# Earlier load and cast of a third weight piece, a gate in the first block, and loads queued ahead of the moves of y, in a recurrence with two MLPs

## The chip, the cores and the metric

The kernel runs on one core of one Trainium2 chip. The metric is the device time in microseconds of one execution; lower is better. The core's engines are TensorE (PE, matmul), VectorE (DVE), ScalarE (ACT), GpSimd (POOL) and SyncE (SP), which here only issues DMAs.

## What is computed

```python
f = 1.0 / (1.0 + np.exp(-f_logit))                  # B 4, H 8, S 768, D 48
for t in range(S):
    state = f[:, :, t, :, None] * state + einsum('bhd,bhe->bhde', k[:, :, t], v[:, :, t])
    y[:, :, t] = einsum('bhd,bhde->bhe', q[:, :, t], state)
x = y.transpose(0, 2, 1, 3).reshape(3072, 384)
x = (sigmoid(x @ w_gate) * (x @ w_val)) @ w_out     # d_ff 1536
h = x @ w_in                                        # d_ff 2048
out = (h * sigmoid(1.702 * h)) @ w_out2
```

All in float32.

## The kernel before

**Three stages that overlap.** The recurrence is cut into 48 units, each of 256 tokens and one pair of heads; four units (numbers 4s to 4s+3) make a step of 256 tokens. The first MLP works on 7 groups of tokens: two of 256 columns, five of 512. Each group has 12 blocks j of 128 hidden columns. The second MLP has 6 groups of 512 with 16 blocks. Every float32 product is made of three matmuls, from a rounded part (hi) and a rest (lo) of each operand: ScalarE's copy makes hi, a subtraction on DVE makes lo. That holds for x (x_hi, x_lo), the hidden activations (act_hi, act_lo) and the weights (w_hi, w_lo).

**What a block does.** PE makes the gate product in `up_ps` bank 0 (`hidden`), then the value product in bank 1, then, where a visit stands, the recurrence's matmuls (`visit`), then the output product of the block before (`out`). ScalarE takes the sigmoid of the gate (L634), DVE multiplies with the value (L823), ScalarE rounds to act_hi (L640), DVE makes act_lo (L832). PE's gate product of block q waits for the sigmoid of block q-1 (`sig_done`), the value product for its mul (`mul_done`).

**Units.** For unit n: SP or ScalarE loads f, SP loads q, k and v. `forget(n)` on ScalarE makes the gates (L545, L546); `prepare(n)` on DVE makes the running product and its inverse (L722, L726); `decay(n)` on POOL makes q_dec (L474) and k_dec (L479). A visit is one turn of PE for up to three units: (turned, kept, made). `turned` gets its scores, `kept` its state update, `made` its y. After it ScalarE copies k and y out of PSUM (`take_k` L564, `take_y` L570), and SP moves y into `x_raw` with two or three DMAs (`move_y` L369). In the blocks from unit 6 on, made = turned - 2.

**Order by hand.** Which block has which visit, gate and prepare is written in tables. In group 0 visits stand at blocks 1, 2, 4, 6, 8, in groups 1 to 5 at 0, 1, 3, 4, 5, 7, 8, 9. Prepares of groups 1 to 5 stand at 0, 2, 3, 4, 6, 7, 10, 11. With a the first turned unit of a group (5 for group 0, 10, 18, 26, 34, 42 for the others), the n-th visit turns unit a+n, and the n-th prepare of a group after 0 is of unit a+n+2. At block 10 (`SPLIT_AT1`) ScalarE runs `x_first_part` for the next group, three casts, one per slab of 128 rows of x (L584), and DVE `x_second_part` (L769). The cast of a slab waits until the y of the units that fill it have been moved (`y_moved`). The third slab needs all units of the group. These are complete with the unit made at block 9. On DVE the prepare at block 10 stands ahead of `x_second_part`.

**Waits of the loads.** `load_f(n)` waits for the gate of unit n-2, `load_kq(n)` for q_dec of n-2 before the two loads of q, and for k_dec of n-2 before those of k. `load_v(n)` waits for the visit that made unit n-4. All SP issues stand in one program, in order.

**Weights of the first MLP.** `load_w1(t)` on ScalarE's queue brings piece t (576 KB) into one of four places, `w1_first_part(t)` is its cast (L526), `w1_second_part(t)` the subtraction on DVE (L776), at block t-2. Piece 0 is split by POOL (L486). Before the first block eight visits have run.

The functions that the change touches, and what calls them:

Of the kernel before, what the change touches and what calls it, by code (L numbers as in the profile page):

```python
# [16 lines left out]
def gla_moe_moe2(nc, q_t, k_t, f_t, v_n, v_t, w1, w2, out_t, x_dram, x2_dram):  # L17
# [51 lines left out]
    ahead_of = VISITS[BEFORE_MLP][0]  # L69
    for g in range(NG1 - 1):  # L70
        if g == 0:
            forgets = {j: n + 3 for n, j in enumerate((1, 2, 4, 6, 8))}
            prepares = {j: n + 1 for n, j in enumerate((0, 1, 3, 5, 7, 9))}
        else:
            forgets = {j: n + 3 for n, j in enumerate((0, 1, 3, 4, 5, 7, 8, 11))}
            prepares = {j: n + 2 for n, j in enumerate((0, 2, 3, 4, 6, 7, 10, 11))}
        FORGET_AT.update({(g, j): ahead_of + n for j, n in forgets.items()})
        PREPARE_AT.update({(g, j): ahead_of + n for j, n in prepares.items()})
        ahead_of += len(forgets)
    SPLIT_AT1 = 10  # L80
    SPLIT_AT2 = 4
    AHEAD = 3
# [1 line left out]
    with ExitStack() as ctx:  # L84
# [9 lines left out]
        def wait(eng, s, value):  # L94

            if value > 0:
                eng.wait_ge(s, value)
# [120 lines left out]
        def pieces_of_pair(p):  # L218

            pieces = []  # L220
            for i in range(PAIR):
                at, end = (PAIR * p + i) * D, (PAIR * p + i + 1) * D
                src = 64 * i
                while at < end:
                    m = min(end, (at // P + 1) * P) - at
                    pieces.append((slice(src, src + m), at // P, slice(at % P, at % P + m)))
                    src, at = src + m, at + m
            return pieces
# [3 lines left out]
        def moves(s, n):  # L232

            return sum(MOVES[m % UG] for m in range(s, n, YS))
# [100 lines left out]
        with nc.Block() as block:  # L335

            @block.sync
            def _(sp):
                def load_f(n):
                    if n < UNITS:  # L340
                        u = Unit(n)
                        sp.wait_ge(gate_done, n - 1)
                        for i in range(PAIR):
                            sp.dma_start(f_raw[rows[i], u.s, :], f_t[u.pair, i, :, u.tokens]).then_inc(f_loaded[u.s], 16)

                def load_kq(n):
                    if n < UNITS:
                        u = Unit(n)
                        wait(sp, q_dec_done, n - 1)
                        for i in range(PAIR):  # L350
                            sp.dma_start(q_raw[rows[i], u.s, :], q_t[u.pair, i, :, u.tokens]).then_inc(q_loaded[u.s], 16)
                        wait(sp, k_dec_done, n - 1)
                        for i in range(PAIR):
                            sp.dma_start(k_raw[rows[i], u.s, :], k_t[u.pair, i, :, u.tokens]).then_inc(k_loaded[u.s], 16)

                def load_v(n):
                    if n < UNITS:
                        u = Unit(n)
                        if n >= 4:
                            sp.wait_ge(visit_done, out_visit[n - 4] + 1)  # L360
                        sp.dma_start(v_raw[:, n % 4, :, :],
                                     v_n[u.pair, :, u.third * BLOCKS:(u.third + 1) * BLOCKS, :]).then_inc(v_loaded[n % 4], 16)

                def move_y(n, pieces=slice(None)):
                    u = Unit(n)
                    sp.wait_ge(y_taken, n + 1)
                    wait(sp, x_split, u.group * KC)
                    for src, slab, dst in pieces_of_pair(u.p)[pieces]:
                        sp.dma_start(x_raw[dst, slab, u.in_group], y_t[src, n % YS, :]).then_inc(y_moved[n % YS], 16)  # L369
# [14 lines left out]
                def load_w2(t):  # L384
                    if t >= STAGED:
                        sp.wait_ge(w2_split, t - STAGED + 1)
                    sp.dma_start(w2_stage[:, t % STAGED, :], w2[:, t * PIECE2:(t + 1) * PIECE2]).then_inc(w2_loaded[t % STAGED], 16)
# [13 lines left out]
                move_y(1)  # L401
                move_y(2, slice(0, 2))
                move_y(3, slice(1, None))
                for n in range(4, 8):
                    load_v(n)
                load_kq(6)
# [3 lines left out]
                for q in range(BLOCKS1):  # L410
                    b = BLOCK[q]
                    if b.j == 1 and b.g:
                        store(b.g - 1)
                    if (b.g, b.j) in VISIT_AT:
                        turned, _, made = VISITS[VISIT_AT[b.g, b.j]]
                        if made is not None:
                            move_y(made)
                            load_v(made + 4)
                        if turned is not None:
                            load_kq(turned + 3)  # L420
                            load_f(turned + 4)
                    if b.g == NG1 - 2 and b.j == J1 - 1:
                        for t in range(STAGED):
                            load_w2(t)
                    if b.g == NG1 - 1 and b.j == 2:
                        load_x2(0)
                        for t in range(STAGED, J2):
                            load_w2(t)
# [86 lines left out]
            def _(act):  # L515
                def load_w1(t):

                    if t >= 4:
                        wait_w1(act, t - 4)
                    act.dma_start(w1_staged(t), w1[:, t * PIECE1:(t + 1) * PIECE1]).then_inc(w1_loaded[t % 4], 16)  # L520

                def w1_first_part(t):

                    act.wait_ge(w1_loaded[t % 4], 16 * (t // 4 + 1))
                    piece = slice(t * PIECE1, (t + 1) * PIECE1)
                    act.copy(w_hi[:, piece], w1_staged(t)).then_inc(w1_hi_done, 1)  # L526
# [8 lines left out]
                def forget(n):  # L535
                    if n >= UNITS:
                        return
                    u = Unit(n)
                    act.wait_ge(f_loaded[u.s], (u.uses + 1) * 32)
                    if n < 2:  # L540
                        act.wait_ge(gaps_set, 5)
                    wait(act, scan_done, n - 1)
                    f_c = f_raw[:, u.s, :].rearrange("p (c t) -> p c t", c=CH)

                    act.activation(gate[:, u.s, :].rearrange("p (c t) -> p c t", c=CH)[:, :, 1:C], f_c[:, :, 1:C], ACT.Sigmoid)  # L545
                    act.activation(floor[:, u.s, :].rearrange("p (c t) -> p c t", c=CH)[:, :, 0], f_c[:, :, 0],  # L546
                                   ACT.Sigmoid).then_inc(gate_done, 1)

                def first_move_y(n, pieces):
                    u = Unit(n)  # L550
                    act.wait_ge(y_taken, n + 1)
                    for src, slab, dst in pieces_of_pair(u.p)[pieces]:
                        act.dma_start(x_raw[dst, slab, u.in_group], y_t[src, n % YS, :]).then_inc(y_moved[n % YS], 16)

                def first_load_f(n):
                    u = Unit(n)
                    wait(act, gate_done, n - 1)
                    for i in range(PAIR):
                        act.dma_start(f_raw[rows[i], u.s, :], f_t[u.pair, i, :, u.tokens]).then_inc(f_loaded[u.s], 16)
# [6 lines left out]
                def take_y(n):  # L566
                    u = Unit(n)
                    act.wait_ge(visit_done, out_visit[n] + 1)
                    wait(act, y_moved[n % YS], 16 * moves(n % YS, n))
                    act.copy(y_t[:, n % YS, :].rearrange("p (c r t) -> p c r t", c=BLOCKS, r=SIDES),  # L570
                             banks(out_visit[n])[:, :, Y_COL:Y_COL + BLOCKS * C].rearrange("p r (c t) -> p c r t", c=BLOCKS)).then_inc(y_taken, 1)
# [36 lines left out]
                forget(4)  # L608
                take_y(1)
                first_load_f(6)  # L610
                forget(5)
                w1_first_part(1)
                take_y(2)
                first_move_y(2, slice(2, None))
                take_y(3)
                first_move_y(3, slice(0, 1))
                first_load_f(7)
                load_w1(2)
                take_k(4)
                x_first_part(0)  # L620
                load_w1(3)
                w1_first_part(2)
                load_w1(4)
                forget(6)
                forget(7)

                for q, b in enumerate(BLOCK):
                    if b.first_mlp:
# [12 lines left out]
                    if b.first_mlp and (b.g, b.j) in VISIT_AT:  # L641
                        turned, _, made = VISITS[VISIT_AT[b.g, b.j]]
# [455 lines left out]
```

## Time and profile before

| | |
|---|---|
| device time, three runs | 968.01, 969.16, 1051.86 us; median 969.16 |
| profiled execution | 968.01 us, its span in the trace 966.2 us |
| granted TensorE clock, mean | 0.992 |
| busy: PE, DVE, ACT, POOL | 98%, 51%, 31%, 11% |

One run in three was far above the other two, which agree within 0.15%. The profiled execution is the fastest one. All rows below are of its span. Times are in microseconds from the span's start unless ns is written. PE's durations overlap, since matmuls are pipelined; the distance from one start to the next is what a matmul costs.

### The profile page before, as it was taken

The page shows a single profiled execution, that of the slowest core. Times are in us where ns is not written, and L with a number is a line of the kernel's source. Part 1 is how long each engine was busy: PE and PEld are TensorE (multiplying, and loading weights), DVE is VectorE, ACT ScalarE, POOL GpSimd, SP SyncE. Part 2 cuts the span into 40 slices and gives each one's busy share as a digit, 9 for nine tenths or more (in the row PEclk, how much of TensorE's full clock was granted, in tenths as well). Part 3 has the DMA queues.
Part 4 walks back from the last instruction along what each step waited for, and adds up shares of the span by engine and source line. Part 5 has one row for each costly group of instructions (what it writes and reads, how often), then busy time and mean ns, then how long its engine had stood idle before and what let it go on. Part 6 is the DMA issues. An engine that isn't in the chain of part 4 may idle for free.

```text
span 966.2 us, 17729 instructions
## 1 busy us (share of the span) xinstructions
PE 948.8 (98%) x7159; PEld 789.7 (82%) x7159; DVE 491.9 (51%) x876; ACT 303.7 (31%) x621; POOL 106.9 (11%) x125
## 2 busy tenths in 40 slices
PE   8899999999999999999999999999999999999997
PEld 5799988888888888888788888888888888888886
DVE  8897876547555664565333234344343443443433
ACT  3453332223222222322224333323332233333322
POOL 4211211101110111111003440000000000000000
PEclk9899999999999999999999999999999999999999
DMA  5652322112111211121022330020020100100000
GB/s 152 204 167 61 83 63 67 53 51 66 52 46 42 82 45 50 33 76 28 24 104 66 98 115 1 0 66 1 1 66 1 55 12 1 66 1 1 33 1 35
DMA packets 44005, 52.33 MB, mean 54 GB/s; under 512 B 8464, under 2 KB 33808, under 8 KB 43920
## 3 DMA queue, kind: packets, MB, share of 16 engines
q1 hardware_dynamic: 41056, 43.20, 15.4%
q10 hardware_dynamic: 2864, 7.95, 2.8%
q8 instruction: 59, 0.97, 0.4%
q14 instruction: 26, 0.21, 0.1%
HBM read 36.96 MB, written 9.44 MB: 48 GB/s over the span
## 4 chain that ended last, share of the span: by engine, by line
PE 90%; DVE 4%; issue 2%; DMA 1%; SPq 1%; ACT 1%; ACTq 0%; POOL 0%; DVEq 0%
PE up_ps L975 16%; PE up_ps L977 16%; PE up_ps L976 16%; PE out_ps L975 12%; PE out_ps L977 11%; PE out_ps L976 11%; PE att_ps L968 3%; PE att_ps L935 2%; PE att_ps L957 1%; DMA stage<-w 1%; PE turn_ps L914 1%; PE att_ps L947 1%; DVE w_lo L776 1%; DMA k_raw<-k_t 1%; DVE act_lo L832 0%
## 5 line engine op out<-in xcount | busy, mean ns | idle before, releaser
L975 PE MATMUL up_ps<-x_hi,w_hi 128*128 128x512 f32 (+1 forms) x792 | 294.2, 372 | 3.6 <-ACT act_f L634 3.0
L977 PE MATMUL up_ps<-x_hi,w_lo 128*128 128x512 f32 (+1 forms) x792 | 293.8, 371 | 0.0
L976 PE MATMUL up_ps<-x_lo,w_hi 128*128 128x512 f32 (+1 forms) x792 | 293.7, 371 | 0.0
L975 PE MATMUL out_ps<-act_hi,w_hi 128*128 128x512 f32 (+1 forms) x540 | 207.9, 385 | 0.7 <-DVE act_lo L832 0.7
L977 PE MATMUL out_ps<-act_hi,w_lo 128*128 128x512 f32 (+1 forms) x540 | 202.9, 376 | 0.0
L976 PE MATMUL out_ps<-act_lo,w_hi 128*128 128x512 f32 (+1 forms) x540 | 202.6, 375 | 0.0
L640 ACT CAST act_hi<-act_f 128x512 fp32r<-128x512 f32 (+1 forms) x180 | 106.5, 592 | 253.0 <-DVE act_f L823 180.7
L832 DVE TENSOR_TENSOR act_lo<-act_f,act_hi 128x512 fp32r<-128x512 f32 (+1 forms) x180 | 118.1, 656 | 113.7 <-ACT act_hi L640 113.7
L975 PEld LDWEIGHTS up_ps<-x_hi,w_hi 128*128 128x128 f32 x792 | 150.0, 189 | 30.0 <-issue 3.6
L976 PEld LDWEIGHTS up_ps<-x_lo,w_hi 128*128 128x128 f32 x792 | 150.1, 190 | 25.3
L977 PEld LDWEIGHTS up_ps<-x_hi,w_lo 128*128 128x128 f32 x792 | 150.1, 189 | 25.2
L826 DVE TENSOR_TENSOR act_f<-act_f,up_ps 128x512 f32<-128x512 f32 x96 | 66.0, 687 | 173.4 <-ACT act_f L636 173.4
L823 DVE TENSOR_TENSOR act_f<-act_f,up_ps 128x512 f32<-128x512 f32 (+1 forms) x84 | 51.1, 608 | 163.0 <-PE up_ps L977 159.5
L975 PEld LDWEIGHTS out_ps<-act_hi,w_hi 128*128 128x128 f32 x540 | 101.6, 188 | 22.2 <-DVE act_lo L832 1.2
L636 ACT ACTIVATE act_f<-up_ps 128x512 f32<-128x512 f32 x96 | 57.4, 598 | 192.9 <-PE up_ps L977 192.9
L977 PEld LDWEIGHTS out_ps<-act_hi,w_lo 128*128 128x128 f32 x540 | 101.6, 188 | 18.7
L976 PEld LDWEIGHTS out_ps<-act_lo,w_hi 128*128 128x128 f32 x540 | 101.7, 188 | 17.3
L634 ACT ACTIVATE act_f<-up_ps 128x512 f32<-128x512 f32 (+1 forms) x84 | 45.0, 535 | 176.8 <-PE up_ps L977 176.8
L726 DVE RECIPROCAL inv_prod<-prod 128x256 f32<-128x256 f32 x48 | 84.1, 1753 | 1.7
L474 POOL TENSOR_TENSOR q_dec<-q_raw,prod 128x256 f32<-128x256 f32 x48 | 35.2, 734 | 317.5 <-DVE prod L722 263.6
L752 DVE SCALAR_TENSOR_TENSOR state<-state,p_end 128x48 f32<-128x48 f32 x176 | 47.4, 269 | 6.2
L479 POOL TENSOR_TENSOR k_dec<-k_raw,inv_prod 128x256 f32<-128x256 f32 x48 | 37.8, 788 | 50.1 <-issue 41.0
(68 smaller groups left out, 511.7 us busy)
## 6 DMA issues: line engine op xcount, KB each, us to landing
stage<-w SPq DMA_DIRECT2D x16, 384.0 KB, 3.2
stage<-w ACTq DMA_DIRECT2D x9, 576.0 KB, 4.4
q_raw<-q_t SPq DMA_DIRECT2D x96, 48.0 KB, 1.9
k_raw<-k_t SPq DMA_DIRECT2D x96, 48.0 KB, 1.9
v_raw<-v_n SPq DMA_DIRECT2D x48, 96.0 KB, 2.2
x_raw<-x_dram SPq DMA_DIRECT2D x6, 768.0 KB, 4.5
out_t<-final SPq DMA_DIRECT2D x18, 256.0 KB, 2.3
f_raw<-f_t SPq DMA_DIRECT2D x80, 48.0 KB, 1.9
```

Source lines behind the costliest of these rows:

```text
L479: pool.tensor_tensor(k_dec[:, u.s, :], k_raw[:, u.s, :], inv_prod[:, u.s, :], ALU.mult).then_inc(k_dec_done, 1)
L634: act.activation(act_f[:, b.t, 0:b.n], up_ps[:, 0, 0:b.n], ACT.Sigmoid).then_inc(sig_done, 1)
L636: act.activation(act_f[:, b.t, 0:b.n], up_ps[:, b.j % 2, 0:b.n], ACT.Sigmoid, scale=1.702).then_inc(sig_done, 1)
L640: act.copy(act_hi[:, b.t, 0:b.n], act_f[:, b.t, 0:b.n]).then_inc(act_hi_done, 1)
L726: dve.reciprocal(inv_prod[:, u.s, :], prod[:, u.s, :]).then_inc(inv_done, 1)
L752: dve.scalar_tensor_tensor(out=after[:, c, :], in0=state_before(u, c), scalar=p_end[:, n, c:c + 1], in1=after[:, c, :], op0=ALU.mult, op1= ...
L823: dve.tensor_tensor(act_f[:, b.t, 0:b.n], act_f[:, b.t, 0:b.n], up_ps[:, 1, 0:b.n], ALU.mult).then_inc(mul_done, 1)
L826: dve.tensor_tensor(act_f[:, b.t, 0:b.n], act_f[:, b.t, 0:b.n], up_ps[:, b.j % 2, 0:b.n], ALU.mult).then_inc(mul_done, 1)
L832: dve.tensor_tensor(act_lo[:, b.t, 0:b.n], act_f[:, b.t, 0:b.n], act_hi[:, b.t, 0:b.n].bitcast(F32), ALU.subtract).then_inc(act_split, 1)
L975: pe.matmul(dst, w_hi[:, at:at + P], m_hi, start=first, stop=False)
L976: pe.matmul(dst, w_hi[:, at:at + P], m_lo, start=False, stop=False)
L977: return pe.matmul(dst, w_lo[:, at:at + P], m_hi, start=False, stop=last)
```

## The change

It does four things. It adds unit 7 to the gates of group 0's blocks (at block 0) and takes it out of the sequence before the first block; the other gates keep their blocks. It issues the load of the third piece of w1 on ScalarE right behind the load of f for unit 6, and casts it before the copy of k of unit 4 (`take_k(4)`) instead of after the casts of x; the cast of the second piece goes behind the copy of y of unit 2. The load of f for unit 7 is issued by SP. And in the blocks SP issues the loads of f and of q and k ahead of the moves of y and the load of v, where it was the other way round.

```diff
-            forgets = {j: n + 3 for n, j in enumerate((1, 2, 4, 6, 8))}
+            forgets = {j: n + 2 for n, j in enumerate((0, 1, 2, 4, 6, 8))}
...
-        ahead_of += len(forgets)
+        ahead_of += 5 if g == 0 else 8
...
                 move_y(3, slice(1, None))
+                load_f(7)
                 for n in range(4, 8):
                     load_v(n)
...
                         turned, _, made = VISITS[VISIT_AT[b.g, b.j]]
+                        if turned is not None:
+                            load_f(turned + 4)
+                            load_kq(turned + 3)
                         if made is not None:
                             move_y(made)
                             load_v(made + 4)
-                        if turned is not None:
-                            load_kq(turned + 3)
-                            load_f(turned + 4)
...
                 first_load_f(6)
+                load_w1(2)
                 forget(5)
-                w1_first_part(1)
                 take_y(2)
                 first_move_y(2, slice(2, None))
+                w1_first_part(1)
                 take_y(3)
                 first_move_y(3, slice(0, 1))
-                first_load_f(7)
-                load_w1(2)
+                w1_first_part(2)
+                load_w1(3)
                 take_k(4)
                 x_first_part(0)
-                load_w1(3)
-                w1_first_part(2)
                 load_w1(4)
                 forget(6)
-                forget(7)
```

## Rows read from the trace of the kernel before

**Rows 1.** The page, busy us, share of the span, instructions by engine.

```profile
PE 948.8 (98%) x7159; PEld 789.7 (82%) x7159; DVE 491.9 (51%) x876; ACT 303.7 (31%) x621; POOL 106.9 (11%) x125
```

**Rows 2.** Stretches: us; busy of PE, PEld, DVE, ACT, POOL; clock, DMA share, GB/s.

```profile
23.00:24.00 1.00, 0.99 (x13) 0.85 (x14) 0.96 (x2) 0.62 (x2) 0.61 (x1) 0.50 0.03 4
...
31.20:34.10 2.90, 0.01 (x1) 0.04 (x1) 0.89 (x4) 2.23 (x6) 0.72 (x1) 0.84 0.99 298
34.10:40.00 5.90, 5.90 (x53) 5.45 (x54) 5.87 (x8) 3.04 (x8) 1.46 (x2) 0.50 0.77 234
...
140.00:470.00 330.00, 327.34 (x3147) 266.47 (x3150) 192.40 (x368) 88.53 (x211) 43.72 (x58) 1.00 0.18 51
```

**Rows 3.** Waits between 27 and 82 us: who for whom, us, times, longest.

```profile
PE up_ps L975 <- ACT act_f L634: 3.0, 1, 3.0
...
DVE act_f L823 <- ACT act_f L634: 2.0, 1, 2.0
```

**Rows 4.** Timelines of ScalarE and DVE at the start: start, duration, instruction [idle before].

```profile
19.41 0.79 ACTq L559 DMA_DIRECT2D f_raw<-f_t  x2
...
26.44 0.45 ACTq L520 DMA_DIRECT2D stage<-w  x1
...
31.72 1.15 ACT L526 CAST w_hi<-stage 128x1152 fp32r<-128x1152 f32 x1 [2.99 <-DMA stage<-w]
...
33.59 0.36 ACT L634 ACTIVATE act_f<-up_ps 128x256 f32<-128x256 f32 x1
...
31.56 0.41 DVE L734 TENSOR_TENSOR scores<-att_ps,causal 128x256 f32<-128x256 f32 x1
```

**Rows 5.** The chain that ended last, 20 to 82 us: start, duration, what.

```profile
34.40 0.51 DVE w_lo L776
...
79.25 0.33 DVE act_f L823
...
79.63 0.38 PE up_ps L975
```

**Rows 6.** Waits of SP's queue, 140 to 480 us, and of ScalarE, 80 to 470.

```profile
SPq L351 <- POOL q_dec L474: 22.5, 3, 7.8
...
ACT gate L545 <- DMA f_raw<-f_t: 7.6, 5, 2.2
```

**Rows 7.** Timeline of the boundary of groups 2 and 3, all engines.

```profile
212.01 1.98 SPq L369 DMA_DIRECT2D x_raw<-y_t  x2
...
219.28 1.66 ACT L584 CAST x_hi<-x_raw 128x512 fp32r<-128x512 f32 x3
...
221.60 0.78 SPq L351 DMA_DIRECT2D q_raw<-q_t  x2
222.05 0.60 ACT L634 ACTIVATE act_f<-up_ps 128x512 f32<-128x512 f32 x1 [1.10 <-PE up_ps L977]
...
223.72 0.78 SPq L354 DMA_DIRECT2D k_raw<-k_t  x2
224.54 0.89 SPq L344 DMA_DIRECT2D f_raw<-f_t  x2
...
225.70 0.39 PE L977 MATMUL out_ps<-act_hi,w_lo 128*128 128x512 f32 x1
225.93 0.39 PE L975 MATMUL up_ps<-x_hi,w_hi 128*128 128x512 f32 x1
```

**Rows 8.** The same of groups 1 and 2.

```profile
131.48 1.16 SPq L369 DMA_DIRECT2D x_raw<-y_t  x2
...
136.59 0.47 PE L975 MATMUL up_ps<-x_hi,w_hi 128*128 128x512 f32 x1 [0.26 <-DVE x_lo L769]
...
137.06 0.78 SPq L354 DMA_DIRECT2D k_raw<-k_t  x2
...
137.63 0.49 PE L975 MATMUL up_ps<-x_hi,w_hi 128*128 128x512 f32 x1
```

**Rows 9.** The page, DMA issues: count, KB each, median us from issue to landing.

```profile
x_raw<-y_t SPq DMA_DIRECT2D x71, 48.0 KB, 2.0
```

## The prediction, on record before the changed kernel was built

> **What bounds the kernel now.** I read the page's busy shares first [rows 1]: PE is busy 98% of the span and DVE 51%, so in most of the run nothing can be won or lost except by making PE stand still. The table of stretches [rows 2] says where PE does stand still: 327.3 of 330 us busy between 140 and 470, at full clock (2.4 GHz), but 0.01 of 2.9 us in 31.2 to 34.1, and in the 5.9 us after that it works all the time at a granted clock of 0.50 (1.2 GHz). So the start holds the one real stall, 3.0 us.
>
> The waits of 27 to 82 us name it [rows 3]. PE waited 3.0 us for ScalarE's sigmoid of block 0 and DVE 2.0 us for the same. ScalarE's timeline [rows 4] shows why: it issued the load of the third piece at 26.44 and stood 3.0 us ahead of its cast, until 31.72; then came the gates of units 6 and 7, and only at 33.59 the sigmoid. PE had by 31.2 ended both products of block 0 [rows 2].
>
> The chain that ended last [rows 5] then says who is the bound behind the stall. From 34.40 to 79.25 it runs on DVE alone (mul, w_lo, act_lo, prod, inverse, states, and "issue"), and goes over to PE at 79.63. In this first group DVE and PE have nearly the same work, and DVE is the later one.
>
> **The change part by part. The start.** The third load is issued behind the load of f for unit 6, at 19.41 + 0.79 = 20.2 instead of 26.44 [rows 4]. DMA then is busy with the second piece, but in 23 to 24 us its share is 0.03 [rows 2], so the third should be in by about 25, at worst 26. That is an estimate: 5.3 us as the same load took before (26.44 to 31.72). Its cast needs 1.15 us and takes the place of idle time, as ScalarE has little to do before the casts of x. The gate of unit 7 goes behind block 0's act_hi, where ScalarE waits for DVE over long stretches. Left ahead of the sigmoid is one gate (0.6 us), so the sigmoid is set by PE's gate product. DVE then comes to block 0's mul when its own earlier work ends, at 31.56 + 0.41 = 32.0 instead of 34.0: 2.0 us, which is its whole idle time before that mul. PE's stall and its half clock go, 3.0 plus about half of 5.9, but since DVE is the bound up to 79 us, PE keeps only DVE's 2.0. The rest comes back as small waits of PE for DVE. **Term 1: -2.0 us.** Bounds: -2.3, if the pauses between DVE's instructions shrink too; and +1.0, if the earlier and the fourth load, now beside the moves of y for units 2 and 3, delay the third slab of x by 3 us (that load took 5.3 us against the 2 us of a move [rows 4, 9]). The load of f for unit 7 goes to SP, 0.9 us in front of four loads of v that are needed 5 us later: nothing.
>
> **Gates and f loads in the blocks.** Only unit 7's gate moves; the later ones keep their blocks. The loads of f and q/k now stand ahead of move_y and load_v. ScalarE waited 7.6 us in five places of 80 to 470 us for f [rows 6], and these waits go. PE waited for none of them: it was busy 327.3 of 330 us [rows 2], and what is left lies in the visits. So this is worth 0.
>
> **What the new order on SP costs.** SP's queue is in order: whatever waits holds what is behind it. So for every visit I asked what load_f(turned + 4) and load_kq(turned + 3) wait for, and whether that comes before the y of the same visit is taken. load_f waits for the gate of unit turned + 2, made in an earlier block in every case. load_kq waits for q_dec and k_dec of unit turned + 1, so for DVE's prepare of that unit. In group 0 the prepares of blocks 0, 1, 3, 5, 7 come before the visits of 1, 2, 4, 6, 8. In groups 1 to 4 all come before too, except one: the visit of block 9 needs the prepare that stands at block **10**. (In group 5 the visit of block 9 has no turned unit.) These are the long waits of SP [rows 6]: 22.5 us in three places of 140 to 480 us, 7.8 at the longest. Today they are harmless, because the move of y and the load of v went out first. After the change the moves of the last unit of the next group stand behind them, and x_first_part, which ScalarE runs at block 10, waits for these moves at its third slab. ScalarE is in order as well: behind it stands the sigmoid of block 11, and PE cannot begin the next group without that.
>
> The boundary of groups 2 and 3 in numbers [rows 7]. Today: the moves at 212.01, x_hi at 219.28, sigmoid of block 11 at 222.05. After: q loads, released by q_dec, at 221.60, k loads, released by k_dec, 223.72 to 224.50. There the f loads stood (224.54), and now the two moves do. The second is issued 0.58 later (two took 1.16 at the other boundary [rows 8]), at 225.12, and lands 2.0 us later [rows 9], at 227.1. The cast of the third slab takes 0.53, the sigmoid 0.60, the signal 0.1: PE can begin at 228.4. Today it begins the next group at 225.93 [rows 7]. Stall: **2.5 us**, between 2.2 and 2.7 for landings of 1.8 to 2.2. The boundaries behind groups 3 and 4 have the same pattern (with this one they are the three waits of [rows 6], about 7.5 us each), so three times: 7.5 us.
>
> The boundary of groups 1 and 2 [rows 8], where blocks are 256 wide and PE is through sooner: k loads from 137.06 to 137.84, moves from 137.88, the second at 138.46, landed at 140.5, cast until 141.0, sigmoid of 256 columns 0.4, PE at 141.5. Today PE starts at 136.59 and, after two short waits for x_lo, runs through from 137.63, its fourth matmul; three take 0.69, so it stands as if started at 136.9. Stall: **4.6 us**, 4.3 to 4.9. **Term 2: 4.6 + 7.5 = +12.1**, bounds 10.9 and 13.0.
>
> **The clock.** The trace has one comparable case: after 3.0 us without a matmul the granted clock was 0.50, and 5.9 us of work ran at it [rows 2], where half was lost: 2.95. For the stall of 4.6 I take these 2.95. For the three of 2.5, shorter than the row, the bounds are 0 and 2.95; I take the middle, 1.5, as the stall is nearer to 3.0 than to the waits of 0.3 that left the clock alone. **Term 3: 2.95 + 3 x 1.5 = +7.5**, bounds 2.95 and 11.8. "TensorE: Matmul & The Clock Gate" of the Trainium skill, section "HAM oscillation — how this bites in real kernels", tells of a kernel in which every wait for a load between two bursts puts the clock back to half. [...]
>
> **Sum:** -2.0 + 12.1 + 7.5 = +17.6 us. The profiled execution took 968.0 (span 966.2), 1.2 below the median of 969.2; the sum gives 985.6 on the one and 986.8 on the other. I say 986.
>
> **Rivals.**
> 1. The stalls are there but the shorter ones leave the clock alone: -2.0 + 12.1 + 2.95 = +13.1, 981. For it: the clock was still full in the first part of the 2.9 us (0.84 in the mean [rows 2]). Chance 0.17.
> 2. All four stalls cost the clock fully: -2.0 + 12.1 + 11.8 = +21.9, 990. Chance 0.15.
> 3. The move isn't held, or comes early enough: then only term 1 is left, 966 to 967, not slower. That would need SP to pass the wait, or PE to have 2.5 us of slack at the boundary; [rows 7] show a matmul every 0.23 us up to 225.93 and none. "DMA: Bandwidth & Descriptors" of the Trainium skill, section "Anatomy of one DMA — SWDGE (gpsimd) path", says that DMA engines don't wait on semaphores and the issuing sequencer does, ahead of dispatch. By that the move can't pass; the rows agree: SP's queue stood 7.8 us for q_dec [rows 6] with nothing passing. Were it otherwise, this rival's 967 would be the result. Chance 0.10.
> 4. The start doesn't win: the x slab is late or the third piece lands after 26.3. Then +1.0 instead of -2.0 and 989 with the rest. It decides if the moves of y for unit 3 land later than about 28, when the third slab is cast today. Chance 0.08.
>
> **How the numbers follow.** Forecast 0.50, rivals as above. Range 974 to 993: below, all low bounds give +9.3 (977), and a little is left for stalls partly hidden; above, rival 2 with the upper bound of the moves, 992. It leaves out rival 3 and a tail. A measurement of this kernel can tell about 2%, 19.4 us, so the line is at 988.5. Over it lie rival 2, most of rival 4 and a tenth of the forecast: 0.27. Faster by over 2% would need a gain that no row has: 0.01. Within: 0.72.
>
> **What the profile after would show.** Right: ScalarE's x_hi at block 10 of groups 1 to 4 with a wait for DMA x_raw<-y_t between the second and third slab, of some 5 to 7 us; PE waits for ScalarE's act_f L634 of about 4.6 once and 2.5 three times; SP's move after the k loads; half clock behind at least the first; at the start no wait for stage<-w, PE's 3.0 gone and DVE's chain at 79 us about 2.0 earlier. Wrong, if the moves go out before the q loads at block 9, if ScalarE's x_hi doesn't wait, or if group 0 gives back much more than 2.0, which would mean that DVE wasn't its bound.

## The result and the profile after

The changed kernel took 981.45 us (median of 6 runs, 980.36 to 983.54) against 969.16 us for the kernel before: a ratio of 1.013, 95% interval 1.0112 to 1.0148. The 969.16 are the median of five runs; a sixth, of 1051.86 us, is a slow one and is left out. The change makes the kernel slower by 1.3%, 12.3 us, where 986 was said. The profiled executions have spans of 966.2 and 980.4 us, 14.2 apart.

The quickest way to see where 14.2 us came in is one instruction that each group has once: ScalarE's first cast of x at block 10. First the kernel before, ScalarE's timeline around the six places (start, duration, instruction, idle before):

```profile
79.92 1.02 ACT L584 CAST x_hi<-x_raw 128x256 fp32r<-128x256 f32 x3
...
132.89 1.75 ACT L584 CAST x_hi<-x_raw 128x512 fp32r<-128x512 f32 x3
...
308.57 1.66 ACT L584 CAST x_hi<-x_raw 128x512 fp32r<-128x512 f32 x3
...
397.85 1.66 ACT L584 CAST x_hi<-x_raw 128x512 fp32r<-128x512 f32 x3
...
486.48 1.66 ACT L584 CAST x_hi<-x_raw 128x512 fp32r<-128x512 f32 x3
```

The one of group 2, at 219.28, stands in [rows 7]. The same of the changed kernel, where the line is L585:

```profile
78.50 1.01 ACT L585 CAST x_hi<-x_raw 128x256 fp32r<-128x256 f32 x3
...
131.48 1.14 ACT L585 CAST x_hi<-x_raw 128x512 fp32r<-128x512 f32 x2
...
139.06 0.62 ACT L585 CAST x_hi<-x_raw 128x512 fp32r<-128x512 f32 x1 [6.45 <-DMA x_raw<-y_t]
...
224.41 1.14 ACT L585 CAST x_hi<-x_raw 128x512 fp32r<-128x512 f32 x2
...
232.34 0.62 ACT L585 CAST x_hi<-x_raw 128x512 fp32r<-128x512 f32 x1 [6.80 <-DMA x_raw<-y_t]
...
317.76 1.14 ACT L585 CAST x_hi<-x_raw 128x512 fp32r<-128x512 f32 x2
...
325.66 0.62 ACT L585 CAST x_hi<-x_raw 128x512 fp32r<-128x512 f32 x1 [6.77 <-issue]
...
409.64 1.14 ACT L585 CAST x_hi<-x_raw 128x512 fp32r<-128x512 f32 x2
...
417.50 0.62 ACT L585 CAST x_hi<-x_raw 128x512 fp32r<-128x512 f32 x1 [6.72 <-DMA x_raw<-y_t]
...
500.79 1.66 ACT L585 CAST x_hi<-x_raw 128x512 fp32r<-128x512 f32 x3
```

Three casts in one piece have become two and one in groups 1 to 4, with 6.5 to 6.8 us between them in which ScalarE waits for a move of y (once the profile names nothing, "issue", but the time is the same). In groups 0 and 5 they are still in one piece. The lead or lag of the first cast over the kernel before is -1.42, -1.41, +5.13, +9.19, +11.79 and +14.31 us. Its steps are what each boundary between two groups cost: 6.54, 4.06, 2.60 and 2.52 us. With the start's -1.42 that is the whole 14.3.

SP's timeline at the boundary of groups 2 and 3 shows the move behind the loads. It answers to [rows 7], where the move went out at 212.01, 7.3 us ahead of the cast:

```profile
226.72 0.78 SPq L351 DMA_DIRECT2D q_raw<-q_t  x2
228.85 0.78 SPq L354 DMA_DIRECT2D k_raw<-k_t  x2
229.72 1.16 SPq L369 DMA_DIRECT2D x_raw<-y_t  x2
230.92 0.58 SPq L361 DMA_DIRECT2D v_raw<-v_n  x1
```

PE's waits in 120 to 420 us are this one row (total, times, longest), where the kernel before had none for the sigmoid:

```profile
PE up_ps L974 <- ACT act_f L633: 11.9, 4, 5.1
```

PE's timeline has the second of the four:

```profile
230.83 0.39 PE L976 MATMUL out_ps<-act_hi,w_lo 128*128 128x512 f32 x1
233.51 0.80 PE L974 MATMUL up_ps<-x_hi,w_hi 128*128 128x512 f32 x1 [2.29 <-ACT act_f L633]
234.11 0.63 PE L975 MATMUL up_ps<-x_lo,w_hi 128*128 128x512 f32 x1
234.53 0.63 PE L976 MATMUL up_ps<-x_hi,w_lo 128*128 128x512 f32 x1
234.96 0.63 PE L974 MATMUL up_ps<-x_hi,w_hi 128*128 128x512 f32 x1
```

Matmuls behind the stall stand 0.43 us apart instead of 0.23: the clock has fallen. The stretches of the four boundaries, each stall and the work behind it (columns as in [rows 2]; the first stall runs from 134.9 to 140.0), say that it did so at two of four. There it fell already within the stall (0.71 and 0.95 in the mean):

```profile
136.00:140.00 4.00, 0.00 (x0) 0.00 (x0) 0.45 (x2) 0.90 (x2) 0.00 (x0) 0.71 0.29 74
140.00:144.00 4.00, 3.99 (x9) 3.14 (x10) 3.49 (x6) 0.82 (x3) 0.73 (x1) 0.50 0.09 25
...
231.20:233.50 2.30, 0.02 (x1) 0.00 (x0) 0.51 (x1) 1.11 (x2) 0.00 (x0) 0.95 0.24 66
233.50:237.00 3.50, 3.49 (x9) 2.77 (x10) 2.78 (x5) 1.03 (x3) 0.61 (x1) 0.55 0.10 25
324.50:326.80 2.30, 0.06 (x1) 0.00 (x0) 0.49 (x1) 1.11 (x2) 0.00 (x0) 1.00 0.24 66
326.80:330.80 4.00, 3.97 (x17) 3.28 (x18) 3.28 (x5) 1.63 (x4) 0.73 (x1) 1.00 0.08 25
416.40:418.70 2.30, 0.08 (x2) 0.04 (x1) 0.55 (x1) 1.11 (x2) 0.00 (x0) 1.00 0.25 70
418.70:422.70 4.00, 4.00 (x18) 3.31 (x19) 3.28 (x5) 1.64 (x4) 0.73 (x1) 1.00 0.11 30
```

The chain that ended last shows the link itself at the last of the four, from the load of k over the move and ScalarE to PE:

```profile
414.43 0.42 SPq L354
...
414.95 0.52 SPq L369
...
415.51 1.96 DMA x_raw<-y_t
...
418.02 0.60 ACT act_f L633
...
418.66 0.50 PE up_ps L974
```

At the start the timelines of ScalarE and DVE answer to [rows 4]:

```profile
25.43 1.15 ACT L527 CAST w_hi<-stage 128x1152 fp32r<-128x1152 f32 x1 [0.88 <-DMA stage<-w]
...
30.89 0.38 ACT L633 ACTIVATE act_f<-up_ps 128x256 f32<-128x256 f32 x1 [1.88 <-PE up_ps L976]
...
32.54 0.42 DVE L822 TENSOR_TENSOR act_f<-act_f,up_ps 128x256 f32<-128x256 f32 x1 [0.70 <-PE up_ps L976]
```

The third piece is cast at 25.43 instead of 31.72, and ScalarE now waits for PE and not PE for ScalarE. DVE still stands 0.70 us, now for PE's value product.

### The profile page after: what moved, and what is told of

The parts are those of the page before. It is cut to its first block, busy times and chain, and to the rows that moved or that the text cites. A ratio compares the mean times of both kernels' runs of the same rounds, so it can differ in the third digit from the quotient of the medians.

```text
span 980.4 us, 17729 instructions
## 1 busy us (share of the span) xinstructions
PE 950.0 (97%) x7159; PEld 789.9 (81%) x7159; DVE 492.6 (50%) x876; ACT 303.4 (31%) x621; POOL 106.8 (11%) x125
## 4 chain that ended last, share of the span: by engine, by line
PE 57%; DVE 0%; DMA 0%; ACT 0%; SPq 0%; issue 0%; ACTq 0%
PE up_ps L974 10%; PE up_ps L976 10%; PE up_ps L975 10%; PE out_ps L974 9%; PE out_ps L976 8%; PE out_ps L975 8%; PE att_ps L967 1%; PE att_ps L934 0%; DMA x_raw<-y_t 0%; PE att_ps L956 0%; PE att_ps L946 0%; PE turn_ps L913 0%; SPq L354 0%; DVE act_lo L831 0%; DVE act_f L825 0%
## 5 line engine op out<-in xcount | busy, mean ns | idle before, releaser
L974 PE MATMUL up_ps<-x_hi,w_hi 128*128 128x512 f32 (+1 forms) x792 | 296.5, 374 | 12.2 <-ACT act_f L633 11.9
```

What stands on the lines that cost most here:

```text
L974: pe.matmul(dst, w_hi[:, at:at + P], m_hi, start=first, stop=False)
```

## The experiments

Each kernel was compared with the kernel before on the same chip. Medians of the kernel before were 969.17 (runs 1 to 4), 969.4 (5 to 8) and 969.23 us (9 and 10).

**1. Only the new order on SP, in the kernel before.**

```diff
+                        if turned is not None:
+                            load_f(turned + 4)
+                            load_kq(turned + 3)
                         if made is not None:
                             move_y(made)
                             load_v(made + 4)
-                        if turned is not None:
-                            load_kq(turned + 3)
-                            load_f(turned + 4)
```

Expected:

> The kernel before with only the new order of SP in the blocks (loads of f, q and k ahead of the moves of y and the load of v). My theory (the moves of the unit made at block 9 are held by the wait for q_dec and k_dec of block 10's prepare): span 966.2 + 15.6 = 981.8, four waits of PE for ScalarE's sigmoid of 4.6 to 5.1 and 2.3 us, and the start's 3.0 us stall as before. Rival A (the loss comes from the start, where DMA and ScalarE are ordered anew): span 966, no wait of PE at the boundaries.

Measured: 984.55 us, ratio 1.016 (1.0145 to 1.0176), span 984.5 of the profiled execution. That is 15.4 us in the medians; the profiled execution is the slowest of the four. PE's waits for the sigmoid at the boundaries are again 11.9 us in four, 5.1 the longest. First casts of x at block 10 are at 81.42, 134.40, 227.46, 320.90, 412.74 and 503.90, so the boundaries cost 6.67, 4.15, 2.56 and 2.53. The whole loss is in the order on SP; rival A falls. The span is 2.7 us above the expected one, and 1.5 of that is the start: DVE's first product with the value stands at 35.47 instead of 33.98, ahead of anything that the edit touches. By so much does the start vary between executions, which is why the small effects below are read from medians.

**2. The changed kernel with the old order in all blocks** (the diff of experiment 1, undone).

Expected:

> The changed kernel with the old order of SP in the blocks, so the start and the moved gate alone. My theory: span 964.8 to 965.0, that is the 1.4 us that the changed kernel had gained by block 10 of group 0, and no wait of PE at the boundaries. Rival A (the start carries the loss): 978 or more.

Measured: 966.87 us, ratio 0.9977 (0.9967 to 0.9987), span 966.8, no wait of PE for a sigmoid at a boundary. The start gains 2.3 us in the medians. In the profile it gained 0.4 (first cast at 79.48), and that span is 1.8 us above the expected one; it is the slowest of the nine executions.

**3. The old order at block 9 alone.**

```diff
+                        late = b.g and b.j == 9
+                        if late and made is not None:
+                            move_y(made)
+                            load_v(made + 4)
                         if turned is not None:
                             load_f(turned + 4)
                             load_kq(turned + 3)
-                        if made is not None:
+                        if not late and made is not None:
                             move_y(made)
                             load_v(made + 4)
```

Expected:

> The changed kernel with the old order (moves of y and load of v first) in one place per group, block 9 of groups 1 to 5, and the new order in all others. My theory: all of the loss goes, span 964.8 to 965.0. Rival B (loads ahead of moves cost something wherever they stand, by later loads of v and later moves): the loss shrinks by less than half, 973 or more, as 4 of 45 visits are changed.

Measured: 967.0 us, ratio 0.9976 (0.9967 to 0.9985), span 965.5. Loads ahead of moves in the other 39 of the 43 visits that turn a unit cost nothing that can be measured; all of the loss stood in four visits. Rival B falls. SP's queue still waits for q_dec in 17 places of 140 to 480 us, 69.3 us in all, without a cost that can be measured.

**4. The prepare of block 10 moved to block 9, SP as changed.**

```diff
-            prepares = {j: n + 2 for n, j in enumerate((0, 2, 3, 4, 6, 7, 10, 11))}
+            prepares = {j: n + 2 for n, j in enumerate((0, 2, 3, 4, 6, 7, 9, 11))}
```

Expected:

> The changed kernel with the seventh prepare of groups 1 to 5 moved from block 10 to block 9 on DVE, SP's order as changed. My theory: q_dec and k_dec come a block earlier, so at the boundaries of the groups of 512 columns the moves go out in time (no stall, each about 8 us earlier), and at that of groups 1 and 2, with blocks of half the width, 1 to 3 us of stall remain: span 965 to 969. Rival C (the moves are late by the number of issues ahead of them, 2.7 us, not by the wait): 979 to 981 as before this edit.

Measured: 969.18 us, ratio 0.9999 (0.9989 to 1.0009), span 968.1. ScalarE's timeline at two boundaries, of 256 and of 512 columns:

```profile
137.16 0.62 ACT L585 CAST x_hi<-x_raw 128x512 fp32r<-128x512 f32 x1 [2.49 <-DMA x_raw<-y_t]
...
311.18 0.62 ACT L585 CAST x_hi<-x_raw 128x512 fp32r<-128x512 f32 x1 [0.32 <-issue]
```

The wait between the casts is 0.3 us where a block takes 8 us and 2.5 where it takes half, and PE has one wait, of 2.3, behind which the granted clock stayed at 1.00. So the moves followed the prepare, not the number of issues ahead of them, and rival C falls. What it still loses lies in group 1 and its boundary: from the first cast of group 0 to that of group 2 it takes 141.1 us (79.35 to 220.44), the kernel before 139.4.

**5. Dummy matmuls in the stalls.** Their product is never read; they keep PE at work while it would stand.

```diff
+                        if 2 <= b.g < NG1 - 1 and b.j == 0:
+                            pe.wait_ge(k_rows_done, VISITS[VISIT_AT[b.g - 1, 9]][0] + 1)
+                            for _ in range(17 if b.g == 2 else 8):
+                                pe.matmul(turn_ps[:, 0:P], ident[:, :], ident[:, :], start=True, stop=True)
```

Expected:

> The changed kernel with dummy matmuls of 128 columns ahead of the first block of groups 2 to 5 (17 ahead of group 2, 8 ahead of the others), which fill the time in which PE waits for the sigmoid; their product is never read. The stalls stay. My theory (part of the cost of a boundary is the half clock behind it): the first two boundaries cost 5.1 and 2.6 us instead of 6.5 and 4.1, the other two 2.6 as before, span 977 to 978, no granted clock of 0.50 behind a boundary. Rival (the boundaries cost what the stall and its late loads cost, the clock adds nothing): span 980 to 981 or more.

Measured: 979.32 us, ratio 1.0101 (1.0086 to 1.0117), span 977.8. Its stretches behind the first two boundaries:

```profile
140.00:144.00 4.00, 3.22 (x14) 2.66 (x15) 3.02 (x5) 2.15 (x6) 0.74 (x1) 1.00 0.12 33
...
230.00:234.00 4.00, 3.48 (x23) 2.99 (x23) 1.66 (x3) 2.13 (x5) 0.00 (x0) 1.00 0.13 39
```

The waits of ScalarE are the same to the hundredth (6.45, 6.80), but first casts at 79.23, 132.24, 223.06, 315.09, 407.07 and 498.23 give boundaries of 4.43, 2.74, 2.70 and 2.53 us. Keeping the clock took 2.1 us off the first and 1.3 off the second, and nothing off the two that had kept it. So of the 15.7 us of the four boundaries in the changed kernel's profile 12.4 are the late moves, and 3.3 were half clock. The dummies did not fill the stalls to the end: PE still waited 2.7 us in four places, 1.3 at the longest.

**6. Only the gate of unit 7 moved, in the kernel before.** Its load of f stays on ScalarE's queue.

```diff
-            forgets = {j: n + 3 for n, j in enumerate((1, 2, 4, 6, 8))}
+            forgets = {j: n + 2 for n, j in enumerate((0, 1, 2, 4, 6, 8))}
...
                 forget(6)
-                forget(7)
```

Expected:

> The kernel before with only the gate of unit 7 moved from ahead of the first block into block 0; its load of f stays on ScalarE's queue. My theory: ScalarE still stands at the third piece until 31.7, so the sigmoid of block 0 comes 0.4 us earlier and no more: stall 2.6 instead of 3.0, first cast of x at block 10 of group 0 at 79.5 instead of 79.9, span 965.5 to 966. Rival (the two gates are what holds the sigmoid): the whole 1.4 us, span 964.8.

Measured: 968.56 us, ratio 0.9993 (0.9984 to 1.0002), span 967.1. ScalarE still stood at the third piece until 31.98 and PE waited 2.8 us for the sigmoid of block 0, not the 2.6 expected. No difference that can be measured. In its profile the first cast of x was at 80.68, later than the 79.5 expected. It sits inside the variation of the start seen in experiment 1.

**7. Only the third piece moved, in the kernel before.** Both gates stay ahead of the first block, in the ScalarE sequence shown in the change.

Expected:

> The kernel before with only the load and the cast of the third piece (and the cast of the second, the load of the fourth) moved; both gates stay ahead of the first block. My theory: the sigmoid of block 0 follows PE's gate product, DVE's wait for it of 2.0 us shrinks to under 1, first cast of x at block 10 of group 0 at 78.5 to 79.5, span 965 to 966. Rival (the gates hold it): less than 0.5 us gained there.

Measured: 967.81 us, ratio 0.9983 (0.9974 to 0.9992), span 965.9, first cast at 79.41. The piece alone gives 1.6 of the 2.3 us of experiment 2. The difference between the two is within the intervals.

**8. Nine dummy products instead of six ahead of unit 4's visit**, on the kernel of experiment 3.

```diff
-                    keep_warm({0: 2, 1: 5, 2: 2, 4: 2, 6: 6, 7: 4}.get(v, 0))
+                    keep_warm({0: 2, 1: 5, 2: 2, 4: 2, 6: 9, 7: 4}.get(v, 0))
```

Expected:

> The version with the old order at block 9 only, and 9 instead of 6 dummy products behind the seventh visit, so that PE does not stand still for up to 2.1 us ahead of the visit that turns unit 4. My theory (in the changed kernel block 0 ran at half clock and DVE waited 0.7 us for its value product): where the clock is full, 0.5 to 0.7 us more gain, span 964 to 965; where it is at half at that point the dummies take twice as long and delay the visit by about 1 us: span 966 to 967. Against that version's 965.5 I expect a difference under 1 us either way.

Measured: 966.77 us, ratio 0.9973 (0.9963 to 0.9984), span 965.1. In its profile block 0 ran at full clock and DVE did not wait for the value product. The dummies did not keep the clock up, though: it fell to 0.50 in 24 to 27 us and was back at 28. Between this and experiment 3 (0.9976) the intervals can't tell.

**9. Only the loads of f ahead of the moves; q and k last, in every block.**

Expected:

> The changed kernel with only the loads of f ahead of the moves of y; those of q and k stand last again, in every block. My theory (load_kq's wait for block 10's prepare is the one harmful wait, load_f's wait is over long before): no stall at the boundaries, 966.5 to 967.5 us as the version with the old order at block 9. Rival (the wait of load_f for a gate, 14.8 us in four places of the changed kernel, also holds moves): one or more stalls of PE for ScalarE's sigmoid stay, 970 or more.

Measured: 967.34 us, ratio 0.9979 (0.997 to 0.9988), span 964.5, all six casts in one piece. SP's queue still waits 6.1 us in three places for a gate, ahead of moves, without harm. So the harmful wait is that of load_kq, and the rival falls.

**10. One of the four places held.**

```diff
-                        late = b.g and b.j == 9
+                        late = b.g not in (0, 3) and b.j == 9
```

Expected:

> The version with the old order at block 9, but with the new order kept at block 9 of group 3, so that one of the four places is held. My theory: one wait of PE for ScalarE's sigmoid of 2.3 us at the boundary of groups 3 and 4, that boundary 2.5 us longer (up to 4.1 if the granted clock falls behind it), all others as without; 967.0 + 2.5 = 969.5 us. Rival (the costs of the four hang together, the first sets off the others): under 1 us.

Measured: 970.77 us, ratio 1.0015 (1.0006 to 1.0024), span 969.7. One wait of PE for the sigmoid, 2.3 us. Its boundary took 4.3 us more than that of experiment 3 (from first cast to first cast 93.59 instead of 89.28 us), and all others what they take without. In the medians this place costs 3.4 us (970.77 against 967.34 in experiment 9, measured on the same chip), more than the 2.5 expected. ScalarE at that boundary:

```profile
307.99 1.14 ACT L589 CAST x_hi<-x_raw 128x512 fp32r<-128x512 f32 x2
...
315.89 0.62 ACT L589 CAST x_hi<-x_raw 128x512 fp32r<-128x512 f32 x1 [6.76 <-issue]
...
401.58 1.66 ACT L589 CAST x_hi<-x_raw 128x512 fp32r<-128x512 f32 x3
```

And the stretch behind it:

```profile
316.00:320.00 4.00, 2.94 (x8) 2.37 (x9) 2.74 (x5) 2.04 (x5) 0.06 (x1) 0.71 0.06 21
```

One held place costs its own share and sets off no other, so the rival falls. The same stall that left the clock alone in the changed kernel's profile at this boundary brought it down here: 2.6 and 4.3 us for one stall.

**The version to keep** is that of experiment 3 or 8, 0.24% to 0.27% faster than the kernel before and 1.5% faster than the changed one.

## Why the prediction came out as it did

**SP's order (term 2, +12.1): right, in place and size.** PE waited 11.9 us in four waits, one of 5.1 and three of 2.3. From these 0.5 has to come off that PE had waited at the first boundary before: 0.26 ahead of its first matmul [rows 8] and as much again ahead of its fourth. The casts of ScalarE stood 6.5 to 6.8 us, where 5 to 7 was said. Experiments 1, 3 and 9 show that the wait of load_kq at block 9 is the cause and the only one; experiment 4 shows that what it waited for is the prepare of block 10. Experiment 10 shows that one held place alone has the same stall. With the clock kept (experiment 5) the four places cost 12.4 us in the profile. In the medians they cost 12.2: 9.9 in experiment 5, and the 2.3 that the start gives back in experiment 2.

**The clock (term 3, +7.5): the mechanism was right, the size more than twice too high.** Experiment 5 puts it at 3.4 us in the profile (2.1 and 1.3), and at 2.4 in the medians (12.3 less 9.9). The first stall was priced at 2.95, from the 5.9 us at half clock of [rows 2], and cost 2.1, as the half clock held for a shorter time behind it: from 140.0 to about 144.5, so 4.5 us. The middle of 1.5 for each of the other three was right only as a mean of two outcomes: one cost 1.3, two cost nothing. Rival 2, all four in full, was further off still (+21.9). Rival 1 (+13.1, the shorter stalls leave the clock alone) came nearest to the measured +12.3, though one of its three stalls did not leave it alone.

**The start (term 1, -2.0): right in size in the medians** (-2.3 in experiment 2, and -1.4 in the profile). That DVE is the bound behind it the traces bear out: from DVE's first product with the value to the first cast of x it takes 45.9 to 46.1 us in eleven of the twelve profiles, among them the kernel before (33.98 to 79.92, with PE's half clock inside) and the changed kernel (32.54 to 78.50). PE's waits moved into group 0 as small ones. In experiment 6 it takes 46.8, which no run explains. The step that erred is that the sigmoid would leave DVE no wait at all. In the changed kernel most of block 0 ran at half clock (0.53 in 30 to 32 us), and DVE waited 0.7 us for the value product. PE had stood 2.1 us ahead of unit 4's visit, but that this brought the clock down is not shown: in experiment 8, where this wait was filled, the clock fell too, only earlier. Experiments 6 and 7 show that the piece carries the gain, the gate none that can be told.

**Loads of f ahead (0): right.** The 7.6 us of ScalarE for f in [rows 6] went with no gain of their own (experiments 2 and 3 are the same).

The sum of +17.6 was too high by 3.4 against the profile (14.2) and by 5.3 against the medians (12.3). In the profile the clock is 4.1 too high, less 0.6 that the start gained less than said and 0.3 that term 2 is short of the 12.4; the rest is rounding and the end of the span. In the medians, -2.3, +12.2 and +2.4 stand against -2.0, +12.1 and +7.5, so all but 0.2 of the miss is the clock. Each of these medians is known to some tenths of a us only, so the split is good to about 1 us.

Why the profile lies above the medians is shown in part. The six executions of the changed kernel spread over 3.2 us. The three longer ones (982.11 to 983.54) had a mean granted clock of 0.989 to 0.991, the three shorter ones (980.36 to 980.8) one of 0.995 to 0.998, and the profiled execution is of the first kind. Where the clock fell in the others isn't known.

The lower end of the range rested on a slip in adding up. The three low bounds are -2.3, +10.9 and +2.95, which is +11.6 and not +9.3, or 981 us and not 977. The measured +12.3 lies just above it.

## What to carry to other kernels

In a queue that issues in order, a load goes behind whatever has an earlier consumer, and what matters is not how long its issue takes but what its semaphore waits for. Check each place of a hand-written table against the step that releases the load: here 39 of 43 visits were safe, and four, where the releasing step stands one block later, cost all of the loss. A wait that has stood in a queue for 7.8 us without harm does harm as soon as something with an earlier consumer is put behind it.

## What the runs showed of the hardware

After stalls of PE of 2.3 us the granted clock fell at some places and not at others, at three of eight in all: in the changed kernel once in three (0.55 behind the boundary of groups 2 and 3, 1.00 behind the next two), once in three in experiment 1 as well (boundaries of 4.15, 2.56 and 2.53), in experiment 10 at a place where it hadn't (0.71 in the mean of 316 to 320), and in experiment 4 not (1.00 from 136 to 144). The stall of 5.1 us brought it down in both profiles that had it without dummy matmuls (boundaries of 6.54 and 6.67). One of 2.8 us, in experiment 6, did not, where the 3.0 us of the kernel before did. A fall behind a boundary cost 1.3 to 2.1 us here. "TensorE: Matmul & The Clock Gate" of the Trainium skill, section "HAM oscillation — how this bites in real kernels", tells of a kernel that falls back in every round, after waits of about 3 to 5 us each. The two stalls of 5.1 us agree with it. The stalls of 2.3 us are shorter than its waits, so it says nothing of them; here three of eight fell. Dummy matmuls in most of the stall kept the clock and gave back 3.4 us in the profile, 2.4 in the medians.
